# Group 0 written by the shared loop body: another order of the peeled first group on VectorE and ScalarE, and another wait on GpSimd

## What is computed

```python
for t in range(S):                       # B, H, S, D = 2, 8, 768, 40
    m_new = max(f_gate[t] + m, i_gate[t])
    f_stab, i_stab = exp(f_gate[t] + m - m_new), exp(i_gate[t] - m_new)
    C = f_stab * C + i_stab * outer(v[t], k[t]);  n = f_stab * n + i_stab * k[t]
    y[t] = sigmoid(o_gate[t]) * (C @ q[t]) / max(abs(n . q[t]), 1)
x = y as 1536 tokens x 320
h = x @ w_in1 (320 x 2048);  x2 = (h - tanh(h)) @ w_out1
h = x2 @ w_in2;              out = (h * tanh(softplus(h))) @ w_out2
```

## Time and profile before

| | |
|---|---|
| median of 3 runs | 436.26 us (435.71 to 445.73) |
| profiled execution, own time | 445.73 us |
| its span, first to last instruction | 443.9 us |
| busy: PE, PEld | 437.3, 424.9 us |
| busy: DVE, ACT, POOL | 267.7, 277.8, 163.5 us |
| granted TensorE clock, mean | 0.999 |

### The profile page before, as it was taken

How to read it: one execution, slowest core, us unless ns; L and a number is a source line. 1 busy time by engine, 2 the same in 40 slices (tenths; PEclk the granted TensorE clock), 3 DMA queues, 4 the chain that set the end, 5 groups by cost and what they waited for, 6 DMA issues and landing times.

```text
span 443.9 us, 9502 instructions
## 1 busy us (share of the span) xinstructions
PE 437.3 (99%) x3501; PEld 424.9 (96%) x3501; DVE 267.7 (60%) x547; ACT 277.8 (63%) x480; POOL 163.5 (37%) x130
## 2 busy tenths in 40 slices
PE   8999998999999999999999999999999999999997
PEld 5889998999999999999999999999999999999996
DVE  5457796659457755944626765767645664575460
ACT  4549637524732652462237579898797779778991
POOL 3148831322422042232218615454422451344243
PEclk9999999999999999999999999999999999999999
DMA  6755150123016002800043140000000000000001
GB/s 214 253 175 183 62 185 0 50 89 113 0 48 197 0 37 73 276 1 1 1 119 89 56 120 1 1 1 32 0 31 0 0 30 0 0 30 2 1 0 61
DMA packets 14861, 28.10 MB, mean 63 GB/s; under 512 B 1584, under 2 KB 7472, under 8 KB 14832
## 3 DMA queue, kind: packets, MB, share of 16 engines
q1 hardware_dynamic: 14444, 26.72, 18.9%
q10 hardware_dynamic: 388, 0.99, 0.7%
HBM read 25.71 MB, written 2.00 MB: 62 GB/s over the span
## 4 chain that ended last, share of the span: by engine, by line
PE 87%; DVE 5%; ACT 4%; issue 2%; POOL 1%; POOLq 1%; ACTq 0%; DVEq 0%
PE bank L1160 38%; PE bank L1168 33%; PE bank L1128 5%; PE bank L1101 3%; PE bank L1113 2%; DVE act_lo L222 1%; PE bank L1144 1%; PE bank L1293 1%; PE bank L1210 1%; PE bank L1138 1%; ACT act_hi L666 1%; DVE act L865 1%; ACT soft L653 1%; ACT soft L658 1%; ACT L658 1%
## 5 line engine op out<-in xcount | busy, mean ns | idle before, releaser
L1160 PE MATMUL bank<-x_lo,wi_hi 128*128 128x256 f32 x528 | 141.8, 283 | 0.0
L1168 PE MATMUL bank<-wo_hi,act_hi 128*128 128x320 f32 x384 | 119.9, 312 | 1.9 <-DVE act_lo L222 1.6
L1168 PE MATMUL bank<-wo_hi,act_lo 128*128 128x320 f32 x384 | 118.6, 309 | 0.0
L1168 PE MATMUL bank<-wo_lo,act_hi 128*128 128x320 f32 x384 | 118.6, 309 | 0.0
L461 POOL TENSOR_TENSOR act_lo<-hid,act_hi 128x512 fp32r<-128x512 f32 x48 | 66.3, 1414 | 98.3 <-ACT act_hi L666 98.3
L1160 PE MATMUL bank<-x_hi,wi_hi 128*128 128x256 f32 x352 | 101.7, 289 | 0.6 <-DVE x_lo L859 0.6
L1160 PEld LDWEIGHTS bank<-x_lo,wi_hi 128*128 128x128 f32 x528 | 101.1, 192 | 0.0
L1160 PE MATMUL bank<-x_hi,wi_lo 128*128 128x256 f32 x352 | 99.6, 283 | 0.0
L222 POOL TENSOR_TENSOR act_lo<-act,act_hi 128x512 fp32r<-128x512 f32 x28 | 36.0, 1287 | 116.7 <-ACT act_hi L525 116.7
L1168 PEld LDWEIGHTS bank<-wo_hi,act_hi 128*128 128x128 f32 x384 | 72.3, 188 | 3.3 <-issue 1.7
L1168 PEld LDWEIGHTS bank<-wo_lo,act_hi 128*128 128x128 f32 x384 | 72.3, 188 | 0.0
(11 more groups left out here) (126 smaller groups left out, 681.5 us busy)
## 6 DMA issues: line engine op xcount, KB each, us to landing
stage<-w_out SPq DMA_DIRECT2D x8, 640.0 KB, 5.5
decay<-neg_top_rows SPq DMA_DIRECT2D x8, 512.0 KB, 3.7
stage<-w_in SPq DMA_DIRECT2D x6, 512.0 KB, 6.1
ks<-k_t SPq DMA_DIRECT2D x12, 160.0 KB
kt<-k_tok SPq DMA_DIRECT2D x6, 320.0 KB, 5.4
out<-out_sb SPq DMA_DIRECT2D x12, 160.0 KB, 1.8
v<-v_tok SPq DMA_DIRECT2D x5, 328.0 KB, 4.8
qs<-q_t SPq DMA_DIRECT2D x10, 160.0 KB
```

Of the source, the lines that this page charges most:

```text
L1160: last = pe.matmul(dst, w, x, start=(n == 0), stop=(n == len(parts) - 1))
L1168: last = pe.matmul(dst[b][:, 0:DM], a[:, t], w[:, j, :], start=(first and n == 0), stop=(last_tile and n == 2))
```

## The change

The two functions `first_group` are gone. Group 0 is now made by the loop body `steps`, which got a parameter on each engine: `splits` on ACT (which weight unit's high part is made in which step) and `first` on DVE. Group 0's instructions are the same ones as before, in another order. On POOL, weight unit 7 waits for `y_ready` 4 (both halves mixed) instead of `state_ready` 4. The orders on PE and SP, the loop and all that follows are unchanged.

```diff
@@ POOL @@
         split_low(pool, 6)
-        pool.wait_ge(state_ready, 4)
+        pool.wait_ge(y_ready, 4)
         split_low(pool, 7)
@@ ACT @@
-        def first_group():
-            tanh(0, 0)
...
-        def steps(g, c, n):
+        def steps(g, c, n, splits=()):
             for k in range(NP):
                 tanh(g, k)
                 if c is not None and k == NP - 1:
                     next_high(c, 0)
+                if k == 0 and splits:
+                    weights_from_rows(c, 0)
                 high_part(g, k)
+                if k == 0 and splits:
+                    weights_from_rows(c, 2)
+                    weights_from_rows(c, 3)
+                for i, step in splits:
+                    if step == k:
+                        split_high(act_, i)
                 if c is None and k < 4:
                     split_high(act_, 8 + k)
-                if c is not None and k == 0:
+                if c is not None and k == (1 if splits else 0):
                     output_gate(c)
                 if n is not None and k == 2:
                     gate_exponentials(n)
...
-        first_group()
+        steps(0, 1, 2, ((3, 1), (4, 1), (5, 2), (6, 3), (7, 4)))
@@ DVE @@
-        def first_group():
-            residue(0, 0)
...
-        def steps(g, c, n):
+        def steps(g, c, n, first=False):
             for k in range(NP):
                 if c is not None and k == 1:
                     weigh_scores(c, 0)
                     weigh_scores(c, 1)
+                if first and k == 1:
+                    low_part(dve, g, 0)
+                    scan_gates(n, 0)
                 residue(g, k)
...
+                if first and k == 0:
+                    carry_column(c)
+                if first and k in (1, 2, 4, 5):
+                    low_part(dve, g, k)
                 if k == 2:
-                    if n is not None:
+                    if n is not None and not first:
                         scan_gates(n, 1)
                     mix(c, 0, False)
                 if k == 3:
                     weigh_scores(c, 2)
                     weigh_scores(c, 3)
+                    if first:
+                        low_part(dve, g, k)
                 if k == 4:
                     mix(c, 1, False)
...
                 if n is not None and k == 6:
                     gate_columns(n, False)
+                    if first:
+                        low_part(dve, g, k)
...
-        first_group()
+        steps(0, 1, 2, True)
```

More of the change, by code:

```diff
@@ L917, in _ @@
         before_loop = links[0]
-        def first_group():
-            residue(0, 0)
[L922 to L934, removed]
-            low_part(dve, 0, 3)
-            residue(0, 4)
-            mix(1, 1, False)
-            low_part(dve, 0, 4)
-            residue(0, 5)
-            update_state(1, 0)
-            update_state(1, 1)
-            low_part(dve, 0, 5)
-            residue(0, 6)
-            gate_columns(2, False)
-            low_part(dve, 0, 6)
-            exponents_of(2, 0)
-            exponents_of(2, 1)
-            residue(0, 7)
-            x_low(score, 0, y_high, 3, x_ready)
-            low_part(dve, 0, 7)
-            x_low(score, 1, y_high, 4, x_ready)
-            carry_column(2)
-            exponents_of(2, 2)
-            exponents_of(2, 3)
-        def steps(g, c, n):
+        def steps(g, c, n, first=False):
             for k in range(NP):
```

## The result

| | before | after |
|---|---|---|
| median of 7 runs | 436.28 us (435.71 to 445.77) | 439.26 us (438.23 to 439.62) |
| profiled execution, own time | 445.73 us | 439.19 us |
| its span | 443.9 us | 437.4 us |
| granted clock, mean | 0.999 | 1.000 |

**The change makes the kernel 0.68% slower: ratio 1.0068, interval 1.0057 to 1.0081**, which is +3.0 us (2.5 to 3.5). Forecast were +3.4 and 439.7.

What follows compares the result with a forecast made beforehand. PE was taken to bound the kernel, with group 0 its only real gap. Walking the new order gave 4.5 - (1.5 - 0.4) = +3.4 us, so 436.26 + 3.4 = 439.7 us; 8 in 10 range 436.9 to 442.9.

Steps and rivals of the forecast that it cites:

- The view that bounded it: Whole kernel: PE busy 437.3 of 443.9 us; only group 0 has a real gap, and full later groups pass shifts on.
- The cause at its root: ScalarE in group 0: five items ahead of tanh 2 make it 6.9 us later, leaving VectorE dry from 41.3 to 45.6.
- the pair: Second pair of score weightings on VectorE in group 0, moved behind residue 3: ends at 53.6, first PE wait 1.6.
- PE's waits: PE in group 0: new waits of 1.6, 0.5, 0.7, 0.8 and 0.8, and about 0.4 ahead of out 7.
- The sum: End of group 0: 4.5 lost up to input tile 7's second half, less (1.5 - 0.4) coming back, +3.4 us.
- signs of being wrong: Group 0: tanh 2 leaving before 43.5, a VectorE instruction with a PSUM input held, or PE waiting for a weight unit.
- PE's chunk sum waits for that pair: PE in group 0: chunk sum of the second half of heads starts at 53.7 instead of 52.07, a 1.6 us wait.
- The scan: VectorE in group 0: moved ahead of residue 1, its second instruction held about 1.2 us by POOL's key weighting.
- the rival with a slower switch: ScalarE table switches ahead of tanh 2 and 3 each hold 1.28 longer; PE's waits grow 1.7, 441.4 us; chance 0.04.
- The rival with the falling clock: Behind PE's new waits the clock drops to 1.2 GHz for 10 us, adding 10 us: 449.7; chance 0.03.
- The rival in which the pair comes in time: Score weightings on VectorE through by 52.0, state update also 1.6 earlier: not slower, 435.0 us; chance 0.08.
- The wait on POOL: POOL's weight unit 7 waiting on y instead of the state gives next to nothing: 0.2 old order, 0.1 new.

Runs made afterwards that it cites:

- the second profile of the kernel before: The kernel before, run once more without any edit to get another trace: 435.95 us, span 434.1.
- the pair's experiment: The changed kernel with the second pair of score weightings put back directly behind residue 2 on VectorE: ratio 1.0068 to the kernel before.
- The experiment without holds: POOL's subtracts of weight units 3 to 7 replaced by zero memsets: changed kernel 435.76 us, 0.9984; kernel before 434.28 us, 0.9954.

## Why the prediction was right

**The view that bounded it** held: PE sets the end, group 0 alone has idle time, and the steady groups pass a shift on unchanged (39.36 busy of 39.36).

**The cause at its root** was right. Tanh 2 was put at 45.0, that is 35.1 on this clock; it ran at 34.91. VectorE's idle time ahead of residue 2 was put at 4.3 and is 4.37. Low part 2 was to be held to 49.0 (39.1) and ended at 38.91; the pair was to end at 53.6 (43.7) and ended at 43.58.

**PE's waits**, in order, forecast and measured: 1.6 and 1.51 for the pair, 0.5 and 0.32 for mix (1,1), 0.7 and 0.44 and 0.8 and 0.71 for the state, 0.8 and 0.53 for the gate columns, 0.4 and 0.42 ahead of out 7. They add up to 4.8 and to 3.93, and the 0.70 more that the trace counts as busy makes up most of the difference. The second half of tile 7 was to start at 68.7 (58.8) and did at 58.49; group 1 was to start at 75.5 (65.6) and did at 65.64.

**The sum** is 3.33 in the trace, for a forecast of 3.4, and this is closer than its terms. Up to the second half of input tile 7, which started at 58.49 instead of 54.26 (64.14 less 9.88), 4.23 were lost where 4.5 were forecast. Behind it 0.89 came back (a wait of 0.42 instead of 1.31) where 1.1 were forecast: the prediction took 1.5 for what the old order lost there, and its own row had 1.31. The two misses, 0.27 and 0.21, nearly cancel, which is luck; the mechanism and the places are not.

None of the signs of being wrong came: tanh 2 didn't leave ahead of 33.6, PE waited for no weight unit, and the second instruction of mix (1,1), which has one input in PSUM, took its 0.50 at 48.14 beside POOL's unit 6.

**What the experiments add.** The prediction put the words "PE's chunk sum waits for that pair" in bold, as if moving the pair were the harm. It isn't: the pair back in its place gives the same time. The order on VectorE and that on ScalarE each cost 1.6 to 2.1 alone. The late tanh 2 alone accounts for 1.2, since high part 2 stays late with the rest. Divided another way, the holds make up about 1.7 and the order without them 1.3.

**Smaller points.** The scan was held for 0.9 (its third instruction took 1.17, and 0.28 in the second profile of the kernel before), where 1.2 on the second instruction was forecast. POOL's key weighting had started later than the walk had it, when its keys landed (26.86, against 36.05 less 9.88), and was shorter (1.33 for 1.72). The table switch cost 1.29 (32.98 to 34.27), and 1.29 again at 38.06, so the rival with a slower switch is out. The trace still doesn't agree with the 2.66 of the Trainium skill's page "ScalarE: Activation LUTs", section "What ACT_TABLE_LOAD costs".

**The other rivals.** The rival with the falling clock came about in part and cost nothing that can be measured: the profile has 1.00 in every window of group 0, through a gap of 1.51, but 15 of the 20 executions have a mean below 1.000, at the same time. Why it cost nothing isn't shown for the change itself; in the pair's experiment 1.5 us lost at the lower level went into waits that PE would have had otherwise. The rival in which the pair comes in time wanted the state update earlier too. The pair's experiment has the first without the second: PE waits for mix (1,1) instead, and nothing is won. The wait on POOL was to give next to nothing, 0.2 in the old order, and the measured 1.0004 agrees with that.

**Left open.** What of the 1.7 us belongs to which hold wasn't tried one by one. The experiment without holds also has shorter units on POOL, so the split of 1.3 and 1.7 is not exact. The 0.70 of busy time was not tried either. At which of its waits the clock of the changed kernel falls, in the executions in which it does, no profile shows.

## What to carry to other kernels

Before moving work in an in-order list, walk the two or three engines through the new order with the durations of the rows, down to where the one that is full next asks for something; it gave each wait of the changed kernel within 0.3 us. The first place at which the full engine waits is not the cause: ask which engine is late as a whole, since repairing that one place moves the wait to the next. And list every wait in the code that names the moved thing, and every instruction that shares the suspected resource, before trusting a walk for a better order: one missed wait and one missed kind of instruction each turned a forecast gain of 2 us into none or a loss.

## What the runs showed of the hardware

- **Holds.** A VectorE instruction with two inputs in SBUF stands while POOL runs a subtract: `tensor_tensor` of 512 columns 0.69 alone and up to 2.00, `scalar_tensor_tensor` (eight of 128 columns) 2.18 alone and 3.98. Beside a POOL memset of the same tiles the low part took 0.68. Even a `tensor_scalar` of 8 columns (L790) took 0.74 at 48.67, beside POOL's unit 6, and 0.17 at 39.89, though it has one input. The Trainium skill's page "SBUF — State Buffer", section "Who interferes with whom", has it so: two SBUF inputs contend with a GpSimd instruction that reads SBUF and not with one that only writes it, and lists `tensor_scalar` among the instructions that can contend. These rows agree.
- **An opening at half rate under a clock of 1.00.** In the first profile of the kernel before (445.73 us) the matmuls of the first 20 us took 0.65 and 1.31 instead of 0.39 and 0.74 in the second (435.95 us), and the span is 9.8 us longer. The granted clock in the record doesn't show it; the length of a known matmul does.
- **The clock behind a gap.** Behind a wait of 3.31 us it was at 0.57 for 3 us, and behind one of 2.15 at 0.50 for 3 us; behind 1.51 in the changed kernel, and behind 1.78 with ScalarE's order alone, it stayed at 1.00 in the profiles. The length of the gap alone doesn't tell: all six executions of the kernel with the gap of 1.78 have a mean clock of 1.000, and 15 of 20 of the changed kernel, whose longest is 1.51 in its profile, have less. An output tile's matmuls stood 0.27 apart at the lower level (32.14, 32.41), against 0.15 at the higher.
